# Attention scores as stacked 128-row products, fed by DMA copies inside SBUF

## The reference

```python
# attention: 4 batches, 8 heads, 768 positions, head size 64
scores = (1 / sqrt(64)) * q @ k.T
keep   = is_sink | in_window            # 4 sinks, window of 128
a      = exp(where(keep, scores, -1e9) - max); a = a / (sum(a) + 1e-9)
x      = a @ v                          # -> 3072 tokens x 512
# dense MLP: w_in 512 x 2048, w_out 2048 x 512
h = x @ w_in; x = (h - tanh(h)) @ w_out
# 8 experts, one a token (argmax of x @ w_gate + bias), 512 -> 1024 -> 512, relu
```

## Time and profile before

| | us |
|---|---|
| median of three runs | 1072.42 |
| the profiled execution's own time | 1070.08 |
| its span, first to last instruction | 1068.1 |
| TensorE busy | 989.9 |
| VectorE busy | 650.4 |
| ScalarE busy | 581.4 |
| GpSimd busy | 327.3 |

### The profile page before, as it was taken

The page is one execution under the profiler, slowest core; times in us unless marked ns, Lnnn a source line. Parts: engine busy times, 40 slices in busy tenths (PEclk is TensorE's granted clock), DMA queues, the critical chain, the costliest instruction groups (busy, mean ns, idle before and its releaser), DMA issues.

```text
span 1068.1 us, 23850 instructions
## 1 busy us (share of the span) xinstructions
PE 989.9 (93%) x7968; PEld 605.0 (57%) x7968; DVE 650.4 (61%) x2272; ACT 581.4 (54%) x1329; POOL 327.3 (31%) x462
## 2 busy tenths in 40 slices
PE   2748999999999999999999999999899999899996
PEld 1524444555554555555455556555487777677774
DVE  6665767667768767777866775646765334633331
ACT  4766786666667765766666675536422224522221
POOL 5766675112116211213511210101032232232322
PEclk9958999999999999999999999999999999999999
DMA  8710001201100320100210010041024211111111
GB/s 315 256 36 19 18 19 66 79 19 35 48 18 19 64 79 19 49 18 19 37 48 19 19 48 1 2 159 59 1 51 174 75 49 54 40 41 49 49 47 40
DMA packets 24375, 60.30 MB, mean 56 GB/s; under 512 B 9504, under 2 KB 9760, under 8 KB 22752
## 3 DMA queue, kind: packets, MB, share of 16 engines
q1 hardware_dynamic: 15392, 45.77, 13.2%
q0 software_dynamic: 5728, 13.43, 4.0%
q10 hardware_dynamic: 3168, 0.02, 0.1%
HBM read 45.35 MB, written 14.12 MB: 56 GB/s over the span
## 4 chain that ended last, share of the span: by engine, by line
PE 73%; DVE 12%; ACT 6%; issue 5%; POOL 1%; DVEq 1%; DMA 1%; ACTq 0%; SPq 0%; POOLq 0%
PE h_ps L751 19%; PE acc L807 18%; PE h_ps L1907 5%; PE s_ps L1856 5%; PE pt_ps L1856 5%; PE acc L1907 5%; PE pt_ps L639 4%; PE s_ps L569 3%; PE x_out L706 3%; ACT probs L587 2%; PE s_ps L858 1%; DVE qk_top L401 1%; PE pt_ps L662 1%; DVE pt_lo L648 1%; PE x_out L1833 1%
## 5 line engine op out<-in xcount | busy, mean ns | idle before, releaser
L807 PE MATMUL acc<-w_out_all,g_hi 128*128 128x512 f16 x768 | 228.4, 379 | 0.0
L751 PE MATMUL h_ps<-xt_hi,w_in_all 128*128 128x384 f16 x960 | 196.8, 328 | 4.2 <-DVE g_raw L772 3.0
L807 PE MATMUL acc<-w_out_all,g_lo 128*128 128x512 f16 x384 | 146.0, 380 | 3.3 <-DVE g_lo L792 2.7
L751 PEld LDWEIGHTS h_ps<-xt_hi,w_in_all 128*128 128x128 f16 x960 | 91.3, 100 | 62.3 <-issue 7.4
L807 PEld LDWEIGHTS acc<-w_out_all,g_hi 128*128 128x128 f16 x768 | 75.1, 98 | 77.7
L763 ACT ACTIVATE g_raw<-h_ps,batch_scale 128x384 f32<-128x384 f32 x120 | 69.5, 579 | 89.2 <-PE h_ps L751 85.3
L792 DVE SCALAR_TENSOR_TENSOR g_lo<-g_raw,batch_scale,g_hi 128x384 f16<-128x384 f32 x128 | 84.6, 661 | 44.4 <-ACT g_hi L782 44.4
L782 ACT ACTIVATE g_hi<-g_raw,batch_scale 128x384 f16<-128x384 f32 x128 | 77.9, 608 | 55.4 <-DVE g_raw L772 54.0
L101 POOL TENSOR_TENSOR tick<-tick 1x1 f32<-1x1 f32 x83 | 15.6, 188 | 293.4 <-ACT y L1923 116.2
L580 DVE CUSTOM_DVE_ANT_0 probs<-s_ps,mask 128x260 f32<-128x260 f32 (+1 forms) x192 | 70.0, 402 | 49.7 <-issue 43.9
L751 PE MATMUL h_ps<-xt_lo,w_in_all 128*128 128x384 f16 x480 | 98.3, 328 | 0.0
(11 more groups left out here) (315 smaller groups left out, 2098.2 us busy)
## 6 DMA issues: line engine op xcount, KB each, us to landing
qk_raw<-in_qk SPq DMA_DIRECT2D x31, 454.0 KB, 3.4
raw<-in_w SPq DMA_DIRECT2D x16, 512.0 KB, 8.1
v_raw<-in_v SPq DMA_DIRECT2D x4, 1536.0 KB, 7.0
x_tokens<-x SPq DMA_DIRECT2D x24, 256.0 KB, 2.5
w_in_all<-in_w_in SPq DMA_DIRECT2D x4, 1024.0 KB, 9.6
w_out_all<-in_w_out SPq DMA_DIRECT2D x4, 1024.0 KB, 9.0
x_tokens<-g_raw SPq DMA_DIRECT2D x1, 1024.0 KB, 12.7
vs_raw<-in_v SPq DMA_DIRECT2D x24, 4.0 KB
```

The source lines that it names most:

```text
L751: mm = eng.matmul(h_of(m, f), w16[0][:, f, x * DM + k * P:x * DM + (k + 1) * P], r[:, par, k, :], start=(i == 0), stop=(i == 3 * KD - 1))
L807: mm = eng.matmul(acc[t][:, :], l[f % 2][:, t * P:(t + 1) * P], w16[1][:, f, x * DM:(x + 1) * DM], start=(f == 0 and i == 0), stop=(f == N ...
```

## The change

From group 5 on (STACKED), each head's scores are two products of 128 rows instead of three of 64. The stationary operand is the head's query, high part on partitions 0 to 63 and low part on 64 to 127. The moving operand is the keys' low part on both halves, then the keys' high part on both halves. The sum therefore also has low x low. The stacked operands are made by twelve DMA copies a group, SBUF to SBUF, 64 partitions each, issued on SyncE's queue (`stack_qk`): 27 groups, 324 copies. They wait for both low parts of the group, and TensorE waits for all twelve before the group's first pair. In `loads` the copies of group g - 2 stand before `load_qk(g)`, and those of the last two groups at the end. For all groups the keys' `conv` moves from i = 6g - 3 to i = 6g - 4, from the odd slot of pair 3g - 2 to its even slot.

```diff
+STACKED = 5
+    q_stack = [sb(f"q_stack{s}", [P, 2, CT], F16) for s in range(2)]
+    kh_stack, kl_stack = ([sb(f"k{x}_stack{s}", [P, 2, KR], F16) for s in range(2)] for x in ("h", "l"))
...
+        def stack_qk(E, eng, g):
+            s = g % 2
+            a = g // HP
+            k = key_cols(a)
+            if E == "sp":
+                eng.wait_ge(q["conv_lo"], 2 * (g + 1))
+                eng.wait_ge(q["scores"], TPC * (g - 1))
+                for hh in range(2):
+                    of_head = slice(D * hh, D * hh + D)
+                    upper, lower = slice(0, D), slice(D, P)
+                    for dst, part in ((q_stack[s][upper, hh, :], q_hi[s][of_head, :]),
+                                      (q_stack[s][lower, hh, :], q_lo[s][of_head, :]),
+                                      (kh_stack[s][upper, hh, k], k_hi[s][of_head, k]),
+                                      (kh_stack[s][lower, hh, k], k_hi[s][of_head, k]),
+                                      (kl_stack[s][upper, hh, k], k_lo[s][of_head, k]),
+                                      (kl_stack[s][lower, hh, k], k_lo[s][of_head, k])):
+                        eng.dma_start(dst, part).then_inc(q[f"stacked{s}"], 16)
+        def stacked(g):
+            return 16 * 12 * ((g - STACKED) // 2 + 1)
...
             if E == "pe":
-                if t == 0:
+                if t == 0 and g < STACKED:
                     eng.wait_ge(q["conv_lo"], 2 * (g + 1))
+                if t == 0 and g >= STACKED:
+                    eng.wait_ge(q[f"stacked{s}"], stacked(g))
...
-                for i, (l, k) in enumerate(((q_lo, k_hi), (q_hi, k_lo), (q_hi, k_hi))):
-                    for j in range(2):
-                        rows = slice(D * (1 - j), D * (2 - j))
-                        mm = eng.matmul(s_banks[j][:, cols], l[s][rows, t * P:(t + 1) * P],
-                                        k[s][rows, t * KB + cols.start:t * KB + KW], start=(i == 0), stop=(i == 2))
+                if g < STACKED:
+                    ...   (the six matmuls as before)
+                else:
+                    for j in range(2):
+                        for i, k in enumerate((kl_stack, kh_stack)):
+                            mm = eng.matmul(s_banks[j][:, cols], q_stack[s][:, 1 - j, t * P:(t + 1) * P],
+                                            k[s][:, 1 - j, t * KB + cols.start:t * KB + KW], start=(i == 0), stop=(i == 1))
...
-                splits = (2, 3) if g == 1 else (6 * g - 5, 6 * g - 3)
+                splits = (2, 3) if g == 1 else (6 * g - 5, 6 * g - 4)
...
             for g in range(4, HP * NC):
+                if g - 2 >= STACKED:
+                    stack_qk("sp", eng, g - 2)
                 load_qk("sp", eng, g)
...
+            stack_qk("sp", eng, HP * NC - 2)
+            stack_qk("sp", eng, HP * NC - 1)
```

More of the change, by code:

```diff
@@ L116, in attention_buffers @@
     pt_hi, pt_lo = (sb(n, [P, 12 + TPC, P], F16) for n in ("pt_hi", "pt_lo"))
-    words = 2 * QK + 2 * CT + 2 * KR + NB2 * DM + 2 * NB2 * HP * VW + 2 * DM + 2 * RING * KW + 6 * KW + 4 * SINK + P + 15 * P
-    return (qk_raw, q_hi, q_lo, k_hi, k_lo, v_raw, v_hi, v_lo, vs_raw, vs_all, probs, normed, sinks, pt_hi, pt_lo), words
+    words = 2 * QK + 4 * CT + 6 * KR + NB2 * DM + 2 * NB2 * HP * VW + 2 * DM + 2 * RING * KW + 6 * KW + 4 * SINK + P + 15 * P
+    return (qk_raw, q_hi, q_lo, k_hi, k_lo, q_stack, kh_stack, kl_stack, v_raw, v_hi, v_lo, vs_raw, vs_all, probs, normed, sinks, pt_hi, pt_lo), words
 def front(nc, dram, shared, attention):
@@ L129, in front @@
         xt_hi, xt_lo = (sb(n, [P, 2, KD, CT], F16) for n in ("xt_hi", "xt_lo"))
-        (qk_raw, q_hi, q_lo, k_hi, k_lo, v_raw, v_hi, v_lo, vs_raw, vs_all, probs, normed, sinks, pt_hi,
+        (qk_raw, q_hi, q_lo, k_hi, k_lo, q_stack, kh_stack, kl_stack, v_raw, v_hi, v_lo, vs_raw, vs_all, probs, normed, sinks, pt_hi,
          pt_lo) = attention
@@ L189, in front @@
         names = ("small_in first_k_in vs_zero v_zero qk_in0 qk_in1 v_in vs_in zero_st fill_st masked "
-                 "qk_scaled qk_mult conv_hi conv_lo sink_zero sink_copied "
+                 "qk_scaled qk_mult stacked0 stacked1 conv_hi conv_lo sink_zero sink_copied "
                  "one_set w_gram top_in top_ps top_out scaled_v scaled_w v_mult v_hi_done v_lo_done vs_mult vs_hi_done vs_lo_done "
@@ L561, in score_pair @@
             if E == "pe":
-                if t == 0:
+                if t == 0 and g < STACKED:
                     eng.wait_ge(q["conv_lo"], 2 * (g + 1))
+                if t == 0 and g >= STACKED:
+                    eng.wait_ge(q[f"stacked{s}"], stacked(g))
                 claim_scores(eng, (q["shifted"], 2 * r + 1))
                 need(eng, q["shifted"], 2 * r)
-                for i, (l, k) in enumerate(((q_lo, k_hi), (q_hi, k_lo), (q_hi, k_hi))):
+                if g < STACKED:
+                    for i, (l, k) in enumerate(((q_lo, k_hi), (q_hi, k_lo), (q_hi, k_hi))):
+                        for j in range(2):
+                            rows = slice(D * (1 - j), D * (2 - j))
+                            mm = eng.matmul(s_banks[j][:, cols], l[s][rows, t * P:(t + 1) * P],
+                                            k[s][rows, t * KB + cols.start:t * KB + KW], start=(i == 0), stop=(i == 2))
+                else:
                     for j in range(2):
-                        rows = slice(D * (1 - j), D * (2 - j))
-                        mm = eng.matmul(s_banks[j][:, cols], l[s][rows, t * P:(t + 1) * P],
-                                        k[s][rows, t * KB + cols.start:t * KB + KW], start=(i == 0), stop=(i == 2))
+                        for i, k in enumerate((kl_stack, kh_stack)):
+                            mm = eng.matmul(s_banks[j][:, cols], q_stack[s][:, 1 - j, t * P:(t + 1) * P],
+                                            k[s][:, 1 - j, t * KB + cols.start:t * KB + KW], start=(i == 0), stop=(i == 1))
                 mm.then_inc(q["scores"], 1)
```

## The result

The kernel before took 1072.43 us (1069.99 to 1073.85), the changed kernel 1078.36 us (1076.60 to 1082.45); the ratio is 1.0059, with a 95% interval from 1.0044 to 1.0075. The change makes the kernel slower by about 6 us. The prediction was "no change that can be told", 1072.4 us with a range to 1077.5: it was wrong, and the time lies outside the range. The profiled execution after took 1078.61 us (span 1076.6); the one before, 1070.08, lay 2.3 us under its median. So the two traces differ by 8.5 us where the medians differ by 5.9.

What follows compares the result with a forecast made beforehand. TensorE was taken to bound the kernel; -6.0 us from shorter score blocks, +3.3 from group 9's copy stall and +2.7 from the moved conversion sum to 0.0, so 1072.4 us, range 1068.0 to 1077.5.

Steps and rivals of the forecast that it cites:

- What bounds the kernel, and the block: TensorE bounds; a pair's score block loses its row-mode gaps, gaining 0.095 or 0.15 us, 6.0 us arriving in all.
- one step more: Rival at the score block: gaps stay or narrow-tile concurrency alone counts; 1087.3 us; chance 0.07 shared with unhidden weights.
- unhidden weights: Rival at the score block: stacked products wait for their own weights, 0.10 us each; 1103 us; chance 0.07 shared with one step more.
- the discounts: Off the 8.4 us gain: 0.6 in window 0, 1.2 in windows 1 to 6, 0.6 for swallowed waits.
- by these the last of twelve lands 11 x 0.44 + 2.1 = 6.9 us after the keys' low part: SyncE's copies: issues of 0.44 us, landing 2.1 after issue; 6.9 us in all, bounds 6.0 and 8.1.
- Hidden by 1.5: Group 7: 8.4 us between the keys' low part and the scores, so the copies cause no wait, with 1.5 us spare.
- Some 0.1 is caught up: Group 9: of TensorE's 3.4 us stall for copies about 0.1 is recovered, leaving a cost of 3.3 us.
- the copies come late in more places: Rival at groups' first pairs: copies outlast the slack in groups 9, 7 and 5; 1076.7 us; chance 0.20, shared with lost clock.
- lost clock: After a TensorE stall of 3.4 us or more, half speed for 3 to 4 us adds about 1.7; within a 0.20 chance.
- moved ahead it adds about 0.5 ... 4 x 0.5: ScalarE's earlier key conversion delays the chain near 301.54 and 326.35 us and 176 us later: 2.0 us in all.
- Where ScalarE has slack that is free: The earlier key conversion, 0.63 us ahead of the MLP's g_hi and the normalisation, costs nothing wherever ScalarE has slack.
- Windows 1 to 6: hidden: There 10.1 us lie between the keys' low part and the scores, the move adding about two; copies cause no wait.

Runs made afterwards that it cites:

- experiment 3: The changed kernel with its twelve copies issued in three steps as parts become ready, four behind the keys' low part: 1072.61 us, ratio 0.9993; +0.6 us by pairs.
- experiment 5: The kernel before with four 128-row products on unstacked parts from group 5, no copies, conversion unmoved, scores not valid: -9.3 us by pairs, 1062.08 us in all.
- experiment 4: The changed kernel with copies issued in three steps and the keys' conversion back in its old odd slot: 1063.67 us, ratio 0.9908.
- experiment 10: The kernel before plus all 324 copies, which nothing reads, conversion unmoved: 1072.98 us, ratio 1.0001.
- experiment 7: The changed kernel with copies in three steps, the keys' conversion in its old slot and group 9 by half rows: 1062.23 us, ratio 0.9912.

## Why the prediction was wrong

The balance in the trace, from pair 14 on: the products -8.0 (experiment 3's +0.6, less the move's 6.9 and its wait of 1.7), the moved conversion +6.9, late copies +9.2. The prediction had -6.0, +2.7 and +3.3. The three add up to the +8.1 measured by construction, since the products' term is what the other two leave, and the split isn't the only one: the products alone bring 9.3 (experiment 5), and with them in place the move costs 8.2 (experiments 3 and 4). If the late copies are taken net (8.4), the products' term is 7.2. So the products' gain is 7.2 to 9.3, the move's cost 6.9 to 8.2, and the late copies' 8.4 to 9.2.

- *What bounds the kernel, and the block.* Right. The gaps belonged to the change between 64 and 128 rows and are gone, and with them the waits for "issue" (81 before, 2 after). The two rivals on the block ("one step more", "unhidden weights") are refuted by experiment 5. The size was low: 7.2 to 9.3 us instead of 6.0, the transposes behind a block being some 0.05 shorter, and the discounts too large.
- *The copies: "by these the last of twelve lands 11 x 0.44 + 2.1 = 6.9 us after the keys' low part"* failed. The slack at group 9 was right (3.5 forecast; 8.93 - 5.48 = 3.45). The twelve took 8.9 us, since an issue costs 0.64 and not 0.44, beyond the bound of 8.1. The value came from a row of 128 partitions from SBUF to DRAM, "nearest in kind"; none of the earlier trace rows was a 64-row DMA from SBUF to SBUF. At group 7 the scores start 144.26 - 133.90 = 10.4 us after the low part: the twelve issues end at 141.78, and the last copy landed 3.0 us after its issue instead of 2.0. "Hidden by 1.5" became a wait of 1.36. Also "Some 0.1 is caught up" was too little: experiments 3 and 4 made up 0.8 of a stall of 1.5 to 1.7.
- *The rival "the copies come late in more places"* is what happened: it was to decide from 8.4 us on, and put 6.0, 1.1 and 0.5 us on groups 9, 7 and 5; measured 5.48, 1.36 and nothing. Its lost clock, 1.7, was 1.4. But the prediction gave it a chance of only 0.20, and its cost was not in the sum.
- *The move: "moved ahead it adds about 0.5 ... 4 x 0.5"* failed, and it is the larger error in kind. Two of the four places cost 1.05 instead of 0.5, since the earlier k_hi also lets k_lo start earlier, into g_lo; two cost 0.3. "Where ScalarE has slack that is free" was wrong at eight more places, 0.2 to 0.7 each, 2.5 us in all. Group 8 cost 1.3 instead of 0.7. With some 0.4 in small steps the sum is 6.9, above the bound of 4. That the move also brings some 1.1 us ahead of pair 14 was not in the forecast either.
- *"Windows 1 to 6: hidden"*: right but for 0.16 us at group 25. *SyncE's queue and the traffic, "nothing"*: right (experiment 10).
- The weight of the errors, by the first split: 5.9 us of late copies beyond the forecast and 4.2 of the move, against 2.0 us more gain, make the 8.1. The medians show 5.9. What lies between is outside the pairs counted: the 1.1 us that the move brings ahead of pair 14 is the part that the traces show, and the rest is not settled.

The cheapest lesson lay in the change itself. It held two costs that served each other, an earlier conversion and twelve copies behind it. Spread the copies over the parts as they become ready, and the earlier conversion is not needed: experiments 4 and 7, 1063.7 and 1062.2 us.

## What to carry to other kernels

When data has to be rearranged between a producer and a tight consumer, issue each transfer as soon as its own part exists, and count the issues behind the last part: here four instead of twelve turned a stall of 5.5 us with its lost clock into one of 1.7. When an instruction moves earlier, follow who starts on its result: the follower moves too, and may now run beside something that it slows. A new kind of DMA has the issue cost of its own kind; without a row of it, let the forecast take the upper bound where the whole gain hangs on a queue of twelve.

## What the runs showed of the hardware

- Back to back on SyncE's queue, DMAs of 64 partitions cost 0.60 us each and 0.04 between, whatever the row length (256 to 2048 B), source or crossing of halves; 128 partitions from DRAM cost 0.43. What makes the difference is open, since 128 partitions from SBUF cost 0.60. Of the 324 copies of the change nine took 1.2 to 1.9 us to issue. A copy from SBUF to SBUF landed after 2.0 us in the median of 324 (1.8 to 3.9).
- A float32 subtraction on VectorE with both tensors in SBUF took 1.13 us instead of 0.62 beside a GpSimd subtraction of 1.18 that had started first and was not lengthened. It goes the other way too: where k_lo started while a g_lo had some 0.45 us still to run, it took 1.49 instead of 1.18 us (group 7 of the change) and 1.25 instead of 0.93 (group 9).
- Behind a stall of 5.5 us the granted clock of 4 us was 0.57, and pair 28 came 6.89 us after pair 27; behind one of 1.7 us the clock stayed at 1.00, and it came after 5.45.
